# A fused attention and gated-channel kernel: the last weight matrix loaded in two transfers by halves of its rows, with a signal each

## The reference

```python
def _moe2_ref(x, w_in, conv_w, w_out):        # x: 2 x 768 x 512, w_in: 512 x 1024
    h = np.maximum(x @ w_in, 0.0)
    ...
    for k in range(K):                        # K = 3, along the 768 positions
        conv_out += conv_w[k][None, None, :] * hp[:, k:k + S, :]
    gate = 1.0 / (1.0 + np.exp(-conv_out))
    return (h * gate @ w_out)                 # w_out: 1024 x 512
```

## Time and profile before

| | us |
|---|---|
| median of 3 runs | 381.51 |
| lowest, highest | 379.96, 382.63 |
| the profiled execution, its own time | 381.0 |
| its span from first to last instruction | 378.9 |
| TensorE busy in the span | 372.1 (98%) |

### The profile page before, as it was taken

One profiled execution on the slowest core, in us unless ns is written; L12 is line 12 of the kernel. 1 busy time (PEld: TensorE's weight loads), 2 busy tenths in 40 slices (PEclk: granted clock), 3 DMA queues, 4 the chain that ended last, 5 costly groups with the idle time before them and its releaser, 6 DMA issues.

```text
span 378.9 us, 6125 instructions
## 1 busy us (share of the span) xinstructions
PE 372.1 (98%) x2166; PEld 328.5 (87%) x2166; DVE 279.4 (74%) x639; ACT 220.1 (58%) x399; POOL 169.1 (45%) x137
## 2 busy tenths in 40 slices
PE   8999999999999999999999999999979999999996
PEld 4799999998888888898888889889768889999996
DVE  5676868665887899999888864347068886989782
ACT  3686868785776786443545173454186779945030
POOL 4999999997345200400000055000199626335720
PEclk9999999999999999999999999999999999999999
DMA  6999879516100353412131341000600000002123
GB/s 204 400 417 385 309 299 330 220 50 246 1 0 3 112 200 134 160 50 83 42 85 42 83 168 55 3 0 2 222 0 0 2 0 0 3 0 85 42 97 112
DMA packets 15760, 43.98 MB, mean 116 GB/s; under 512 B 4464, under 2 KB 5744, under 8 KB 15728
## 3 DMA queue, kind: packets, MB, share of 16 engines
q1 hardware_dynamic: 15728, 43.57, 32.1%
HBM read 32.16 MB, written 11.40 MB: 115 GB/s over the span
## 4 chain that ended last, share of the span: by engine, by line
PE 92%; DMA 4%; SPq 1%; DVE 1%; issue 1%; ACT 1%
PE bank L636 32%; PE bank L798 19%; PE bank L872 15%; PE bank L686 9%; PE bank L669 5%; PE bank L655 4%; PE bank L778 3%; DMA wo<-w_out_in 2%; DMA qk_sb<-qk_laid 2%; PE bank L697 1%; PE bank L811 1%; SPq L321 1%; DVE biased L1370 0%; ACT bank L1155 0%; ACT bop L1195 0%
## 5 line engine op out<-in xcount | busy, mean ns | idle before, releaser
L798 PE MATMUL bank<-b_ops,a_ops 128*128 128x512 f32 x324 | 75.5, 391 | 0.0
L798 PEld LDWEIGHTS bank<-b_ops,a_ops 128*128 128x128 f32 x324 | 60.5, 188 | 12.3
L636 PE MATMUL bank<-v_span,win 128*128 128x512 f32 x288 | 66.7, 391 | 2.2 <-ACT h_sb L1144 2.2
L636 PEld LDWEIGHTS bank<-v_span,win 128*128 128x128 f32 x288 | 53.7, 188 | 13.7 <-ACT h_sb L1144 2.6
L572 POOL TENSOR_TENSOR win<-winraw,win 128x1024 fp32r<-128x1024 f32 x4 | 9.6, 2404 | 69.7 <-ACT win L1078 69.7
L872 PE MATMUL bank<-bop,a_place 128*128 128x384 f32 x160 | 40.6, 334 | 0.0
L947 ACT ACTIVATE pT<-bank 128x512 f32<-128x512 f32 (+1 forms) x48 | 26.8, 558 | 18.5 <-PE bank L686 17.4
L636 PE MATMUL bank<-wth,xT 128*128 128x512 f32 x144 | 35.9, 399 | 0.0
L636 PE MATMUL bank<-uT,wch 128*128 128x384 f32 x192 | 34.8, 336 | 0.0
L636 PEld LDWEIGHTS bank<-uT,wch 128*128 128x128 f32 x192 | 33.8, 188 | 0.6
L686 PE MATMUL bank<-v_sb,pT 128*128 128x65 f32 x264 | 33.7, 269 | 0.0
(11 more groups left out here) (128 smaller groups left out, 745.0 us busy)
## 6 DMA issues: line engine op xcount, KB each, us to landing
qk_sb<-qk_laid SPq DMA_DIRECT2D x7, 792.0 KB, 10.1
w_raw<-w_tok_laid SPq DMA_DIRECT2D x6, 768.0 KB, 11.2
a_kept<-stage SPq DMA_DIRECT2D x6, 768.0 KB, 4.8
a_ops<-a_kept SPq DMA_DIRECT2D x6, 768.0 KB, 4.9
v_sb<-v_laid SPq DMA_DIRECT2D x5, 780.0 KB, 7.7
a_kept<-stage SPq DMA_DIRECT2D x9, 384.0 KB, 3.5
a_ops<-a_kept SPq DMA_DIRECT2D x9, 384.0 KB, 3.1
out<-acc SPq DMA_DIRECT2D x6, 384.0 KB, 2.4
```

Of the source, the lines that this page charges most:

```text
L636: last = pe.matmul(dst, w[a], m[b], start=(i == 0 and j == 0), stop=(i == n - 1 and j == 2))
L798: last = pe.matmul(y_bank(s)[:], a_ops[:, slot, hi, blk, :], b_ops[:, side, blk, lo, :], start=(blk == 0 and j == 0), stop=(blk == NT - 1 ...
```

## The change

The single DMA of `wo` becomes two, issued one behind the other by SP. The first carries row blocks 0 to 3 (A11 and A21, 1 MB) and signals `wo_in`; the second carries row blocks 4 to 7 (A12 and A22, 1 MB) and signals a new semaphore, `wo_second`. `high_a(0)` on ACT still waits for `wo_in`, which now stands for the first half alone; it reads A11, which lies in that half. The first sum on POOL, which reads A21 and A22, waits for both signals. No other instruction is added, taken away or moved on any engine.

```diff
+            w_out_rows = w_out.rearrange("(f p) n -> p f n", p=P)
-            sp.dma_start(wo[:], w_out.rearrange("(f p) n -> p f n", p=P)).then_inc(wo_in, 16)
+            sp.dma_start(wo[:, 0:HF, :], w_out_rows[:, 0:HF, :]).then_inc(wo_in, 16)
+            sp.dma_start(wo[:, HF:FB, :], w_out_rows[:, HF:FB, :]).then_inc(wo_second, 16)
...
             def sum_w_out(n, dst, a, b, op, after):
                 if n == 0:
                     pool.wait_ge(wo_in, 16)
+                    pool.wait_ge(wo_second, 16)
```

More of the change, by code:

```diff
@@ L187, in build @@
             h_ready h_relu pads_ready tap_ready conv_step conv_ready sig_ready g_ready g_hi g_lo wo_in
-            wo_sums a_high a_low b_high b_pool b_dve first_done second_done staged_b out_ready out_copied out_summed stored0""".split()
+            wo_second wo_sums a_high a_low b_high b_pool b_dve first_done second_done staged_b out_ready out_copied out_summed stored0""".split()
         (
@@ L196, in build @@
             u_hi, u_lo, mix_ready, v_ready, v_hi, v_lo, h_ready, h_relu, pads_ready, tap_ready, conv_step,
-            conv_ready, sig_ready, g_ready, g_hi, g_lo, wo_in, wo_sums, a_high, a_low, b_high, b_pool, b_dve,
+            conv_ready, sig_ready, g_ready, g_hi, g_lo, wo_in, wo_second, wo_sums, a_high, a_low, b_high, b_pool, b_dve,
             first_done, second_done, staged_b, out_ready, out_copied, out_summed, stored0
```

## The result

The changed kernel takes 378.50 us (median of 8 runs, 378.15 to 378.70) against 381.26 for the kernel before (8 runs, 379.96 to 382.65): a ratio of 0.9915, 95% interval 0.9893 to 0.9937. That is 2.8 us or 0.85% less, clear of the scatter and under the 1% that the prediction named. The prediction expected a change of this size to read as no difference; the interval excludes that. Two things stand out: the gain is 0.6 us larger than the 2.2 forecast, and the eight times of the changed kernel lie within 0.55 us, those of before within 2.7.

The account below looks back on a forecast made before the run. TensorE, busy for 372.1 of 378.9 us, was taken to bound the kernel. Nothing removed, the 2.18 us gap closed and additions at nothing sum to -2.18 us, from the median 381.51 to 379.3 us; range 377.8 to 381.7.

Parts of the forecast that it names:

- The bound and the place of the cost: PE bounds, with only 6.8 us of the span not its own; the load costs one PE gap of 2.18 us.
- The way by ACT's list: `high_a(0)` waits 6.76 us on ACT, holding `relu(8)` behind it, which PE's `hidden(9)` needs; early release closes the 2.18 us gap.
- The landing of the first half: First 1 MB of `wo` lands 5.1 us after its issue, at 269.3; bounds 4.9 and 9.3 us.
- the pair of `w_raw`: Two neighbouring 768 KB loads landing in 5.0 and 7.3 us, taken to show the earlier is served first.
- the latest harmless landing: PE's gap closes fully if the first half lands by 271.3, up to 7.1 us after the issue.
- The order of the two transfers: The first `wo` transfer is served before the second, freeing ACT early; the 2.2 us gain hangs on this.
- (a): Both halves of `wo` are served together, the first landing at 9.3 us: no gain, 381.5 us; chance 0.07.
- (c): Halves alternate with split overhead; ACT's first signal comes up to 0.6 us later: 382.1, at most 382.4 us; chance 0.05.
- `relu(10)` and what is late next: On ACT, `relu(10)` ends 8.5 us behind the landing, at 277.8, 2.1 us early for PE's `hidden(11)`.
- The second landing and POOL: Second half of `wo` lands about 0.6 us later, at 274.1; POOL's waits cover it, so it costs nothing.
- The sum: Whole kernel: 0 - 2.18 (PE's gap) + 0 = -2.18 us, to 379.3 us.

Follow-up runs that it names:

- the serial kernel: Changed kernel with ACT's first rounding waiting for both signals and SP issuing the second transfer only after the first has landed: 383.37 us, ratio 1.0068.
- the first experiment: Changed kernel, both transfers kept, but ACT's first rounding waits for both signals: 382.73 us, ratio 1.002.
- experiment 180: Not a separate run: the first experiment, where 180 counts PE matmuls; changed kernel with ACT's first rounding waiting for both signals, 382.73 us.
- the last run: The kernel before, unchanged, run once more for a second trace and more times: 381.11 us (12 runs).

## Why the prediction was right

**The bound and the place of the cost**: right. PE's gap of 2.18 us was all that the load cost beside what hangs on a gap; both traces of before and the serial kernel give the time back as 378.5 + gap + 0.3, with 1.6 more where the clock fell. The bound of 6.8 us takes PE's busy time as fixed, which it is only while the clock stays: in the first experiment 180 of its matmuls took 1.57 us more.

**The way by ACT's list**: right, and shown from two sides. With the early half but without its use (both signals awaited) nothing is gained; without the early half but with the list reordered everything is.

**The landing of the first half**: mis-sized, within its bounds. The forecast took 5.1 us from `wchraw`; it was 5.9 with the second transfer behind it (5.8 and 5.6 in two of the experiments), and 5.0 when that was held back. So a second transfer does slow the first, by 0.4 to 0.9 us. The forecast took from the pair of `w_raw` the order alone; its first member already took 5.0 us for 768 KB, nearly the 5.1 of `wchraw` for 1024 KB. The room of 2 us up to the latest harmless landing took this in. That point (7.1 us) was sound: 6.8 us gave no gap, 7.6 us one of 0.45, where 7.6 - 7.1 is 0.5.

**The order of the two transfers**: as forecast. 5.9 us against 9.7 leaves no place for rivals (a) and (c). The Trainium skill's ring order (DMA: Bandwidth & Descriptors, "Queues, rings and completion order") agrees with all traces in which ACT waited for the first transfer alone: it landed at 3.6 us for 512 KB, 5.9 for 1 MB, 6.8 for 1.5 MB and 7.6 for 1.75 MB, and the last of the load at 9.1 to 9.7 us after the first issue. The Trainium skill's rule on two transfers (the same page, "Rules for kernel authors"), which the prediction draws on, is about halves of the partitions; both transfers here cover all 128 partitions, so no run tests it.

**`relu(10)` and what is late next**: right, 8.5 us behind the start of `a_first` (269.90 to 278.42), and early by 1.4 us. The earlier release with A11 alone gains nothing, so nothing else hung on ACT.

**The second landing and POOL**: the split's price, forecast as 0.6 us, was 0.4 between the two traces (9.7 against 9.3). That isn't resolved, since the single load took 8.4, 9.3 and 9.4 us in three traces. It was hidden as forecast, with POOL back in step at 301.40.

**The sum**: -2.18 us, measured -2.76 between the medians, -2.85 between the profiled executions. Of the latter 2.18 are the gap, 0.33 the restart behind it, and 0.16 a start that happened to be earlier (246.94 against 246.78, as above); the remaining 0.18 lies outside this stretch. What the sum left out is the restart, and the clock: in 19 of the 52 executions of before in the two series (7 of 17, 9 of 23, and 3 of 12 in the last run) the mean clock was 0.994 to 0.996 and the time 382.1 to 383.9 us, the others were 379.8 to 381.8. Taken evenly, 1.6 us in 19 of 52 are 0.6 us per execution. That is a share of the mean and not a term between the medians: in the measurement of the result three of before's eight times lie at 382.4 to 382.7 (their clocks aren't on record), the median falls between the groups, and the means differ by 2.89 us (381.37 against 378.48). The prediction has no term for the clock; its one trace shows a granted clock of 1.00 before, in and behind the gap. That before's upper group is the half clock behind this gap is argued from its mean clock and times, which are those of the first experiment's upper group; the fall itself was seen in traces of that kernel and of the serial one alone. The means of before's two groups are 2.0 us apart (380.75 and 382.71), 0.4 more than the clock's 1.57; that the load landed later in the upper group would explain it, and no trace shows it.

**Where luck came in**: the 2.18 us are the gap of one execution. With the other traced execution of before the same sum would have given -1.30 us. Against the changed kernel the lower group of before is slower by 2.3 us on the mean, gap and restart together, so a forecast of 2.2 comes near it partly because a long gap stood in for the restart that was left out.

## What to carry to other kernels

Look behind a wait, not only at it: an engine that runs its list in order passes a wait on to all that stands behind, and here moving one instruction down the list was worth as much as splitting the load. The price of a late load is the gap that it leaves on the bounding engine, with a little more for what hangs on a gap; it is read from that engine's timeline and is here far shorter than the DMA's step in the chain (2.18 against 9.29 us); once it was closed, a still earlier signal bought nothing. A gap read from one trace is one execution's gap: take a second trace before you price it. Where single times of a kernel spread over more than its changed version's, look at the mean granted clock of each execution before calling it noise.

## What the runs showed of the hardware

- After a rest of 2.51 and of 3.14 us TensorE took up its work at full clock and fell to 1.2 GHz 0.4 to 1 us later, for a little over 3 us, which cost 1.6 us in either case (42.70 and 42.71 us for matmuls that took 41.13). After rests of 2.18, 1.30, 0.63 and 0.45 us the traces show none. Whether it falls differs between executions of one kernel; counted by the mean clock (0.991 to 0.996 against 0.999 or 1.0), with the gap of the one trace beside it, it fell in 8 of 12 with a gap of 2.51, in 6 of 6 with 3.14, in none of 12 with 0.63.
- A gap in TensorE's stream cost about 0.3 us beyond its length at full clock (68.65 against 68.32 us for the same 312 matmuls, and 0.76 us in all for a gap of 0.45).
- A DMA of 2 MB in pieces of 2 KB took 8.4 us in one execution and 9.3 in another of the same kernel. 1 MB took 5.0 to 5.2 alone and 5.6 to 5.9 with a second MB queued behind it; 1.5 MB took 6.8 and 1.75 MB 7.6 with the rest behind them.
